# Placing the last-batch rows of the first expert by products with a slot table, in a fused attention + two-MoE kernel

## The reference

```
# 2 batches x 8 heads, 1152 keys, queries averaged in pairs: 576 per head
attn = softmax(scale * q_pool @ k.T) @ v            # -> x, 1152 tokens x 512
# first MoE, 8 experts, 1024 hidden, capacity 288
expert_idx = argmax(x @ w_gate); gate_w = its probability
for i in tokens:                                     # in token order
    e = expert_idx[i]
    if counts[e] < capacity:
        disp[e, counts[e]] = x[i]; pos[i] = counts[e]; counts[e] += 1
y = relu(disp @ w1) @ w2;  out[i] = gate_w[i] * y[expert_idx[i], pos[i]]
# second MoE: 8 normalisations of P = exp(logits) over rows and columns, then
out += P[:, e] * (relu(x @ w1[e]) @ w2[e])           # for every e
```

## Time and profile before

| | |
|---|---|
| time, median of 3 runs | 1270.71 us (1270.53 to 1270.99) |
| time of the profiled execution | 1271.21 us |
| span of the profiled execution | 1269.5 us |
| mean granted TensorE clock | 0.993 |
| busy: PE, PEld, DVE, ACT, POOL | 98%, 92%, 55%, 43%, 51% |
| chain that ended last | PE 95%, ACT 2%, POOL 1%, DVE 1% |

### The profile page before, as it was taken

The page is one execution under the profiler, slowest core; times in us unless marked ns, Lnnn a source line. Parts: engine busy times, 40 slices in busy tenths (PEclk is TensorE's granted clock), DMA queues, the critical chain, the costliest instruction groups (busy, mean ns, idle before and its releaser), DMA issues.

```text
span 1269.5 us, 22823 instructions
## 1 busy us (share of the span) xinstructions
PE 1247.7 (98%) x8084; PEld 1162.9 (92%) x8084; DVE 700.6 (55%) x1587; ACT 549.5 (43%) x1225; POOL 646.9 (51%) x531
## 2 busy tenths in 40 slices
PE   8999999969999999999999999999999999999998
PEld 7999999959999999988988988998998998998996
DVE  7999999952222221786654544544543543543552
ACT  7777887766665552422312412412421422322320
POOL 7655568349888664554343443433532532533512
PEclk9999999979999999999999999999999999999999
DMA  4364433146776531111112111111111011110001
GB/s 127 120 205 140 142 103 129 65 143 232 185 187 188 183 129 67 35 34 67 34 34 67 33 46 53 33 66 33 33 66 33 33 66 33 34 65 33 33 0 69
DMA packets 72450, 107.24 MB, mean 84 GB/s; under 512 B 7206, under 2 KB 38758, under 8 KB 72384
## 3 DMA queue, kind: packets, MB, share of 16 engines
q1 hardware_dynamic: 67792, 97.29, 23.6%
q10 hardware_dynamic: 2816, 4.72, 2.2%
q0 software_dynamic: 1776, 4.37, 0.9%
HBM read 94.92 MB, written 11.81 MB: 84 GB/s over the span
## 4 chain that ended last, share of the span: by engine, by line
PE 95%; ACT 2%; POOL 1%; DVE 1%; issue 0%; DMA 0%; POOLq 0%; DVEq 0%; ACTq 0%
PE psum L1704 31%; PE psum L1751 26%; PE psum L1634 8%; PE psum L1617 6%; PE psum L1458 6%; PE psum L1491 6%; PE psum L1469 6%; PE psum L1693 2%; PE psum L1509 1%; ACT wsplit L710 1%; POOL wsplit L583 1%; PE psum L1606 1%; POOL wsplit L578 0%; PE psum L1561 0%; PE psum L1578 0%
## 5 line engine op out<-in xcount | busy, mean ns | idle before, releaser
L1704 PE MATMUL psum<-wsplit,acts 128*128 128x512 f32 x1728 | 396.6, 390 | 0.0
L1704 PEld LDWEIGHTS psum<-wsplit,acts 128*128 128x128 f32 x1728 | 322.9, 188 | 66.3
L1751 PE MATMUL psum<-acts,wsplit 128*128 128x288 f32 x1800 | 260.9, 295 | 0.0
L1751 PEld LDWEIGHTS psum<-acts,wsplit 128*128 128x128 f32 x1800 | 247.2, 188 | 1.1
L667 POOL TENSOR_TENSOR wsplit<-raw,wsplit 128x512 fp32r<-128x512 f32 x64 | 86.0, 1367 | 296.8 <-ACT wsplit L710 296.8
L1419 DVE SCALAR_TENSOR_TENSOR x<-psum,eqr,x 128x512 f32<-128x512 f32 x126 | 94.6, 751 | 234.1 <-PE psum L1704 234.1
L657 POOL TENSOR_TENSOR wsplit<-raw,wsplit 128x512 fp32r<-128x512 f32 x109 | 140.1, 1326 | 139.3 <-ACT wsplit L710 139.3
L960 ACT ACTIVATE acts<-psum 128x288 fp32r<-128x288 f32 x240 | 92.3, 411 | 193.2 <-DVE psum L1385 118.3
L710 ACT ACTIVATE wsplit<-raw 128x512 fp32r<-128x512 f32 x301 | 169.5, 622 | 0.4 <-PE psum L1634 0.3
L710 ACT ACTIVATE acts<-psum 128x384 fp32r<-128x384 f32 (+2 forms) x304 | 119.0, 448 | 101.2 <-PE psum L1634 56.0
L967 ACT ACTIVATE raw<-psum 128x288 f32<-128x288 f32 x60 | 24.5, 408 | 298.7 <-PE psum L1751 298.7
(11 more groups left out here) (171 smaller groups left out, 1449.6 us busy)
## 6 DMA issues: line engine op xcount, KB each, us to landing
raw<-in_moe_w_dram SPq DMA_DIRECT2D x32, 1024.0 KB, 5.3
raw<-in_moe_w_dram SPq DMA_DIRECT2D x64, 512.0 KB, 4.2
raw<-in_k_dram SPq DMA_DIRECT2D x15, 576.0 KB, 3.7
raw<-in_q_dram SPq DMA_DIRECT2D x15, 576.0 KB
raw<-in_v_dram SPq DMA_DIRECT2D x16, 288.0 KB, 4.5
slots_in<-zero SPq DMA_DIRECT2D x3, 1536.0 KB, 8.7
x<-slots_in ACTq DMA_DIRECT2D x7, 576.0 KB, 6.9
out_dram<-zero SPq DMA_DIRECT2D x3, 768.0 KB, 6.6
```

Source lines behind the costliest of these rows:

```text
L1704: last = mm(psum[:, bank, :], hs[a][:, l, tile * P:(tile + 1) * P], w2f[z][:, l, :], start=(l == 0 and (a, z) == (0, 0)), stop=(l == LF - ...
L1751: last = mm(psum[:, bank, 0:QN], w1f[a][:, x, cc, i * P:(i + 1) * P], src(z, cc), start=(not adds and cc == 0 and (a, z) == (0, 0)), stop= ...
```

## The change

The way to the first expert is rearranged.

- The rows of expert 0 that came from the first batch are loaded from `slots_in` early in the last head (`d0row`; unfilled slots are zero). TensorE turns them by products with the identity (`early_rows`), which open an accumulation in banks 4 to 7.
- The last batch's rows of expert 0 no longer go through DRAM. `first_slots` on DVE compares each token's slot number with a table of 0 to 287 (`slotid`, made by POOL), which gives a 0/1 matrix `hot` per tile. `late_rows_hi` on ACT and `late_rows_lo` on DVE make the scaled rows as two rounded parts, and TensorE adds (tile part).T @ hot for 5 tiles, 2 parts and 4 column parts (`place_late`): 40 products of 288 columns. The result is what `dt_evac` reads.
- The scatters of the last batch remain, for the later experts. They come later: their rows are scaled by ACT (`scale_rows`) after four `hi_w1` pieces (tiles 0, 1) and after `dt_evac` (tiles 2 to 4). The load of expert 1's rows moves from ACT's queue to SP's, behind the landing of all scatters.
- Of expert 0's w1, POOL makes the first half in the last head, both parts (`hi_w1` is new on POOL). ACT and DVE make the second half. The planes of `raw` are renumbered for it, and SP's order of loads changes.
- `slot_limit` and `scatter_index` run once for both last groups, and `expert_starts` and `owner_index` after `dt_evac`.

```diff
@@ block.sync @@
-            load_w2(0, 0, 0)
+            load_w1(0, 0, 0)
+            sp.wait_ge(scattered, 16 * QT)
+            sp.dma_start(d0row, slots_in[0:CAP, :].rearrange("(t p) d -> p t d", p=SR)).then_inc(d0_loaded, 16)
             sp.wait_ge(pt_ready, SCH * G)
-            load_w1(0, 0, 0)
+            load_w1(0, 0, 1)
             sp.wait_ge(vs_done, 2 * G)
             sp.wait_ge(misc_ready, G + 1)
-            load_w1(0, 0, 1)
-
-            sp.wait_ge(scattered, 16 * RT)
-            for c in (1, 3):
-                sp.dma_start(drow[0][:, :, c * P:(c + 1) * P],
-                             slots_in[0:CAP, c * P:(c + 1) * P].rearrange("(t p) d -> p t d", p=SR))\
-                  .then_inc(d0_loaded[c], 16)
-            sp.wait_ge(d0_loaded[3], 16)
+            load_w2(0, 0, 0)
+            sp.wait_ge(idx_done, 2)
             load_w2(0, 0, 1)
...
-            for e in range(1, 6):
+            load_expert(0, 1, 1, (0,))
+            sp.wait_ge(scattered, 16 * RT)
+            sp.wait_ge(dt_ready, DC)
+            sp.dma_start(drow[1], slots_in[CAP:2 * CAP, :].rearrange("(t p) d -> p t d", p=SR)).then_inc(d_loaded, 16)
+            load_expert(0, 1, 1, (1, 2, 3))
+            for e in range(2, 6):
@@ block.gpsimd @@
-            scatter_rows(1, *GROUPS[1])
-            scatter_rows(2, *GROUPS[2])
-            for f in range(FC):
+            for f in range(FC // 2):
+                hi_w1(0, f)
                 lo_w1(0, f)
+            pool.wait_ge(pt_ready, SCH * G)
+            pool.iota(slotid, pattern=[[1, CAP]], base=0, channel_multiplier=0,
+                      allow_small_or_imprecise_dtypes=True).then_inc(slotid_done, 1)
+            pool.wait_ge(d0_loaded, 16)
+            scatter_rows(1, QT, RT)
+            pool.wait_ge(lo_done, FC)
@@ block.scalar @@
+            def late_rows_hi(group):
                 act.wait_ge(gate_done, group + 1)
                 act.wait_ge(x_done, G + group - 1)
                 for n in range(*GROUPS[group]):
                     t = n - QT
+                    nc.scalar.activation(late[0][0:qw(t), t, :], x[0:qw(t), t, DM:2 * DM], ACT.Copy,
+                                         scale=gate[0:qw(t), n:n + 1]).then_inc(late_hi, 1)
...
-            for f in range(FC):
+            act.wait_ge(hi_done, FC // 2)
+            for f in range(FC // 2, FC):
                 hi_w1(0, f)
-            for f in range(FC // 2):
-                hi_w2(0, f)
+            scale_rows(1)
...
             for c in range(DC):
                 dt_evac(0, c)
-            for f in range(FC // 2, FC):
+            scale_rows(2)
+            for f in range(FC):
                 hi_w2(0, f)
@@ block.vector @@
+            def first_slots(b):
...
+                for n in range(*GROUPS[b]):
+                    w = qw(n - QT)
+                    nc.vector.tensor_scalar(hot[0:w, n - QT, :], slotid[0:w, :], pos[0:w, n:n + 1], None,
+                                            ALU.is_equal).then_inc(hot_done, 1)
+            def late_rows_lo():
+                dve.wait_ge(gate_done, 3)
+                dve.wait_ge(pv_ready, 2 * G)
+                for n in range(QT, RT):
+                    w, t = qw(n - QT), n - QT
+                    dve.wait_ge(late_hi, t + 1)
+                    nc.vector.scalar_tensor_tensor(late[1][0:w, t, :], x[0:w, t, DM:2 * DM], gate[0:w, n:n + 1],
+                                                   late[0][0:w, t, :].bitcast(F32), ALU.mult,
+                                                   ALU.subtract).then_inc(late_lo, 1)
...
-                slot_limit(b)
                 slot_number(b)
-                scatter_index(b)
-            expert_starts()
-            owner_index()
+                first_slots(b)
+            slot_limit(1)
+            scatter_index(1)
+            late_rows_lo()
+            experts_held()
+            for f in range(FC // 2, FC // 2 + 2):
+                lo_w1(f)
@@ block.tensor @@
+            for c in range(DC - 1):
+                early_rows(c)
             prefix(2)
+            early_rows(DC - 1)
+            pe.wait_ge(late_hi, 2)
+            pe.wait_ge(hot_done, 2)
+            for c in range(DC):
+                place_late(0, c, 0, 2)
+            pe.wait_ge(pos_read, 2)
             totals()
+            pe.wait_ge(late_hi, QT)
+            pe.wait_ge(hot_done, QT)
+            for c in range(DC):
+                place_late(0, c, 2, QT)
+            pe.wait_ge(late_lo, 2)
+            for c in range(DC):
+                place_late(1, c, 0, 2)
+            pe.wait_ge(late_lo, QT)
+            for c in range(DC):
+                place_late(1, c, 2, QT).then_inc(dt_ready, 1)
```

More of the change, by code:

```diff
@@ L101, in build_attention_moe_moe @@
                 .rearrange("p (j n) -> p j n", j=KJ) for i in (0, 1)] for r in (0, 1)]
+        late = [acts[:, at:at + QT * DM].rearrange("p (t d) -> p t d", t=QT) for at in (QT * CAP, 2 * KJ * GW[0])]
+        hot = acts[:, 0:QT * CAP].rearrange("p (t n) -> p t n", t=QT)
+        assert QT * CAP + QT * DM <= 2 * KJ * GW[0] and QT * DM <= 2 * KJ * GW[1]
         qs = [[acts[:, PTB + (2 * u + i) * QP:PTB + (2 * u + i + 1) * QP] for i in (0, 1)] for u in (0, 1)]
@@ L119, in build_attention_moe_moe @@
         lt = small[0:2 * LO, 0:N]
+        slotid = small[:, 0:CAP]
         assert N <= S
@@ L271, in build_attention_moe_moe @@
         yx_done = sem("yx_done")
-        d0_loaded = [sem(f"d0_loaded{c}") for c in range(DC)]
+        d0_loaded = sem("d0_loaded")
+        slotid_done = sem("slotid_done")
+        hot_done = sem("hot_done")
+        late_hi = sem("late_hi")
+        late_lo = sem("late_lo")
         dt_ready = sem("dt_ready")
@@ L779, in scale_rows @@
             def scale_rows(group):
+                act.wait_ge(late_lo, GROUPS[group][1] - QT)
+                for n in range(*GROUPS[group]):
+                    t = n - QT
+                    part = x[0:qw(t), t, DM:2 * DM]
+                    nc.scalar.activation(part, part, ACT.Copy, scale=gate[0:qw(t), n:n + 1]).then_inc(scaled_act, 1)
+            def late_rows_hi(group):
                 act.wait_ge(gate_done, group + 1)
@@ L1243, in _ @@
                 dt_evac(0, c)
+            for f in range(FC // 2 + 2, FC):
+                lo_w1(f)
+            expert_starts()
+            owner_index()
             for e in range(E):
@@ L1593, in totals, with early_rows, place_late @@
                 last.then_inc(tot_ready, 1)
[L1595 to L1604 removed]
+            def early_rows(c):
+                pe.wait_ge(d0_loaded, 16)
+                for t in range(ST):
+                    mm(psum[:, BDT + c, t * SR:(t + 1) * SR], d0row[:, t, c * P:(c + 1) * P], ident[0:SR, 0:SR],
+                       start=(t == 0), stop=False)
+            def place_late(i, c, a, z):
+                for t in range(a, z):
+                    last = mm(psum[:, BDT + c, 0:CAP], late[i][0:qw(t), t, c * P:(c + 1) * P], hot[0:qw(t), t, :],
+                              start=False, stop=(i == 1 and t == QT - 1))
+                return last
+            for c in range(DC - 1):
+                early_rows(c)
+            prefix(2)
+            early_rows(DC - 1)
[4 more added lines that the diff above has]
+            pe.wait_ge(pos_read, 2)
+            totals()
+            pe.wait_ge(late_hi, QT)
[8 more added lines that the diff above has]
+                place_late(1, c, 2, QT).then_inc(dt_ready, 1)
+            def turn_rows(e, c):
+                if c == 0:
+                    pe.wait_ge(d_loaded, 16 * e)
+                pe.wait_ge(dt_done, DC * e + c)
                 for t in range(ST):
```

72 lines of the change are left out of this document (36 added, 36 removed).

## The result

The changed kernel took 1272.53 us (median of 22 executions: 21 of them 1271.61 to 1275.03, and one of 2501.56 that nothing here explains). The kernel before took 1270.82 us on the same chip (median of 22, 1269.96 to 1271.44). The ratio is 1.0016, interval 1.001 to 1.0022. Forecast were 1264.3 us and a range of 1262.2 to 1267.8. The change is no gain: the time is 8.2 us over the forecast.

A forecast was written before the change was run, and what follows sets the result against it. TensorE, busy 98%, was taken as the bound, so only its waits, slow clock and own instructions count. 6.6 + 0.3 - 0.5 = 6.4 us off 1271.21 gives 1264.8, as median 1264.3; range 1262.2 to 1267.8.

The forecast's parts named there:

- The last head: POOL's copies and subtractions there, 7.4 us, 8 with hand-overs, end near 252.5; hidden, neighbour's cost taken as nothing.
- group 1: ACT's two high parts replace two scalings; DVE's two `hot` of 0.30 replace 0.6 of small steps: no cost.
- the identity products: Nine on TensorE ahead of the prefix count, 0.21 us each, 1.9 in all, ending at 272.3.
- TensorE's placing: 40 products at 0.134 us; the last 12 end at 279.7, expert 0's first hidden product near 280.1, 4.0 us earlier.
- w1's second half of expert 1 ... I take 0.4: Load queued behind expert 1's rows, issued 286.4, landing 292.7; ACT wants it at 291.1; cost 0.4 us.
- I take 1.00 throughout: Granted clock stays at 1.00 (2.4 GHz), as TensorE no longer has a gap over 0.5 us.
- The waits in the hidden products: TensorE waits for DVE's low part of block 0 after expert 0's first 48 hidden products; 0.8 us lost.
- The one that ended slower: Expert 1's rows land late behind ten scatters on SP; TensorE idles 7.2 us, clock costs 3.4 more; 1275; chance 0.06.
- DVE slowed by POOL: DVE's low parts and weight parts take 2.0 us more; gain 4.4, 1266.3; chance 0.12.
- The clock falling by the sparse products: Identity products use few columns, waits are scattered; clock falls anyway, 3.6 us lost; gain 2.8, 1267.9; chance 0.10.
- The clock's part: Slow clock's share, priced at 3.4 us, of cutting expert 0's hidden part from 16.3 to 12.8 us.
- 6.6 + 0.3 - 0.5: Earlier end of expert 0's hidden products, plus projection waiting removed, less 0.5 taken off: 6.4 us gain.

The follow-up runs named there:

- e3_both: Changed kernel, with expert 1's second w1 half issued before SP's scatter wait and the 64-row placing products grouped last; 1265.21 us, 0.9956 of before.
- e5_pad128: Changed kernel with expert 1's second w1 half loaded early and the 64-row tile's placing products made 128 rows high, old order; 1264.77 us, 0.9952 of before.
- e7_split_late: As e3_both, but POOL splits its half of w1 after the slot table instead of in the last head; 1272.19 us, 1.0010 of before.
- e1_load_early: Changed kernel with the second half of expert 1's w1 issued on SP before the wait for the scatters; 1266.77 us, 0.9969 of before.
- e4_before_warm: Kernel before, plus 38 unread products of ones with zeros in TensorE's gap before the first transpose; 1270.28 us, 0.9998 of before.
- e2_group64: Changed kernel with the 64-row tile's placing products grouped after those of the 128-row tiles; 1269.84 us, 0.9992 of before.

## Why the prediction was wrong, point by point

- **The last head, group 1, the identity products, the count: right.** Nine identity products, 18 records, took 2.19 us with the tail of the last (forecast 0.21 a product), and the placing with the slot table began at 272.90, 0.6 us ahead of the forecast. `hot` took 0.65 for two and 0.92 for three; the low parts 3.39 for five, ending at 277.6 (forecast 277.9). POOL's split in the last head, 243.97 to 251.7, left DVE's rows as they were: three low parts (L1044, L1019 before) took 1.48 us with and without it.
- **TensorE's placing: the first step that failed.** It has "40 x 0.134" and "the last 12 follow: 279.7", with the pace of a row of products all 128 rows high, and no cost for the fifth tile's 64 rows. It ended at 282.0: the last 32 took 7.45 us, where that pace gives 4.3. In e3_both, with the 64-row products apart, the hidden products started at 280.71, and in e5_pad128 at 279.90. Mis-sized by 1.9 us at that place, 2.2 at the end of the hidden products (about 295.9 instead of 293.7).
- **"w1's second half of expert 1 ... I take 0.4": the second step that failed, and the dearer one.** The place was named and the queue was right; the size was 3.8. The issue came 3.1 us later than forecast, of which 2.3 is the placing carried on through `dt_evac`, the scalings and the scatters and the rest the first scatter's 1.34 and the waits between; the landing took 7.0 instead of 6.3. The forecast saw that `h_evac(5)` to `(7)` were queued behind the piece, but not that `dt_evac` of expert 1 was too, for which TensorE waits before the second group of transposes.
- **"I take 1.00 throughout": failed in that wait.** From 295.87, where the transposes start, to 315.29 are 19.4 us; less 3.8 of waiting 15.6, where 14.1 was forecast: 1.5 us of slow clock. 2.2 + 3.4 (3.8 less the 0.4 that was in the forecast) + 1.5 = 7.1 us, against 7.0 from 308.3 to 315.29. So the two steps and the clock account for the profiled execution. The median is 0.8 us above it, and no trace shows where the longer executions lose that. e3_both, which mends both, took 1265.21, within the range forecast for the change.
- **The waits in the hidden products: right**, 0.73 against 0.8.
- **The rivals.** The one that ended slower had the right queue, SP behind ten scatters, and the right second price, the clock. It named the row load, which landed in 4.6 us and was in time, and not the weight load behind it. Once the weight load is moved ahead, the row load is what TensorE waits for, as the rival had it: 1.29 us in e5_pad128. DVE slowed by POOL: not in the changed kernel, shown in e7_split_late. The clock falling by the sparse products: not in its profiled execution. In e1_load_early's it fell, but in the slow placing and not in the identity products that the rival names. That would fit the changed kernel's executions with a lower mean clock, which have no trace.
- **The gain as a sum.** The clock's part was 2.4 us and not 3.4, and in e4_before_warm 1.1 of it came through alone. In e3_both the hidden part ran at 1.00 throughout and ended at 294.57, 5.8 us earlier than before, where 6.6 were forecast. In the sum "6.6 + 0.3 - 0.5" only 0.4 of the 0.5 has a source.

## What to carry to other kernels

When work fills a gap, follow each queue that now starts behind the filled-in work, one step further than the wait that is looked for: a delay of 2.3 us on TensorE came back through ACT, POOL and SP as 3.8 us of waiting and 1.5 of slow clock. A load that depends on nothing should not stand behind a wait for something else on its queue; but when it goes ahead, look at what is in flight beside it: the scatters then landed 2.7 us later in e3_both. Products of another row count go in a row of their own, or are padded, and a small DVE instruction with two SBUF inputs should be ordered ahead of a long unbroken row of POOL's, by a wait if need be.

## What the hardware showed that was not expected

- A change between 128-row and 64-row products costs about 0.2 us each way, an estimate from the triples: 0.79 us for a triple instead of 0.40, in the changed kernel. All 128 high, the same 32 products took 4.89 instead of 7.45 us.
- A DVE instruction of 128x10 with SBUF inputs took 15.16 us beside twelve subtractions of POOL that followed each other, and 0.17 us with one wait on POOL.
- With 1 MB of weights issued ahead, the last scatter had landed 5.0 us after its start (e3_both) instead of 2.3 (e2_group64), taken by the time at which SP issues the load behind it.
- The granted clock fell to 0.50 in e1_load_early's profiled execution from about 278 on, while TensorE's products counted as busy without a break but its weight loads filled only 1.24 of 2 us. With 1.23 of 2 us in the same window of the changed kernel's trace it stayed at 1.00.
